# Second mixture: value products one block later, joins ahead of the copies, weight loads two at a time

## What is computed

```python
logits = x @ w_gate                      # x: 2304 tokens of 512
expert_idx = np.argmax(logits, axis=1)
gate_w = softmax(logits)[np.arange(N), expert_idx]
for e in range(E):                       # E = 8, hidden size F = 1024
    mask = expert_idx == e
    h = np.maximum(x[mask] @ w1[e], 0.0)
    out[mask] = gate_w[mask, None] * (h @ w2[e])
```

## Times and profile before

| | us |
|---|---|
| runs shown | 1200.71, 1200.39, 1196.43 |
| median | 1200.39 |
| profiled execution, its time | 1200.34 |
| its span in the trace | 1198.7 |
| PE busy | 1127.6 (94% of the span) |
| DVE busy | 591.6 (49%) |
| ACT busy | 289.2 (24%) |
| POOL busy | 311.6 (26%) |

### The profile page before, as it was taken

One profiled execution on the slowest core, in us unless ns is written; L12 is line 12 of the kernel. 1 busy time (PEld: TensorE's weight loads), 2 busy tenths in 40 slices (PEclk: granted clock), 3 DMA queues, 4 the chain that ended last, 5 costly groups with the idle time before them and its releaser, 6 DMA issues.

```text
span 1198.7 us, 19280 instructions
## 1 busy us (share of the span) xinstructions
PE 1127.6 (94%) x6726; PEld 984.0 (82%) x6726; DVE 591.6 (49%) x1158; ACT 289.2 (24%) x429; POOL 311.6 (26%) x191
## 2 busy tenths in 40 slices
PE   9999999999999999999999999999998889768874
PEld 6889988999999999999999998887776668656753
DVE  6345443222222222222232688885565877767764
ACT  3454334321111131111132111114501210221210
POOL 7200000510000060000033000016685640674640
PEclk9999999999999999999999999999998989888988
DMA  9233213300000120000031011117358734764844
GB/s 341 71 106 94 72 44 98 123 18 0 0 0 0 51 89 0 0 0 0 0 101 40 28 27 26 26 27 240 113 143 174 224 100 89 186 160 114 224 96 85
DMA packets 113315, 99.79 MB, mean 83 GB/s; under 512 B 72559, under 2 KB 97263, under 8 KB 113138
## 3 DMA queue, kind: packets, MB, share of 16 engines
q1 hardware_dynamic: 92498, 62.35, 20.8%
q10 hardware_dynamic: 16272, 25.21, 6.5%
q0 software_dynamic: 4496, 11.56, 3.2%
HBM read 73.48 MB, written 10.92 MB: 70 GB/s over the span
## 4 chain that ended last, share of the span: by engine, by line
PE 75%; DMA 9%; DVE 9%; issue 3%; SPq 2%; DVEq 1%; ACT 0%; POOL 0%; POOLq 0%
PE psum L1364 12%; PE psum L1366 12%; PE psum L1365 12%; PE psum L1410 11%; PE psum L1411 11%; PE psum L1412 11%; DMA h_planes_T<-h_planes 8%; DVE h_row_T L1181 2%; DVE h_planes L1173 2%; PE psum L1600 1%; DVE hThi L1191 1%; PE psum L1601 1%; PE psum L1602 1%; DVE psum L1183 1%; PE psum L1292 1%
## 5 line engine op out<-in xcount | busy, mean ns | idle before, releaser
L469 POOL TENSOR_TENSOR weights_r<-weights,weights_r 128x1024 fp32r<-128x1024 f32 x96 | 232.3, 2445 | 629.6 <-ACT weights_r L658 628.4
L1364 PE MATMUL psum<-xhi,weights_r 128*128 128x384 f32 (+1 forms) x772 | 260.0, 337 | 0.0
L1366 PE MATMUL psum<-xhi,weights_r 128*128 128x384 f32 (+1 forms) x772 | 257.8, 334 | 0.0
L1365 PE MATMUL psum<-xlo,weights_r 128*128 128x384 f32 (+1 forms) x772 | 257.7, 334 | 0.0
L1410 PE MATMUL psum<-weights_r,hhi 128*128 128x512 f32 x576 | 226.9, 394 | 0.0
L1412 PE MATMUL psum<-weights_r,hlo 128*128 128x512 f32 x576 | 224.8, 390 | 0.0
L1411 PE MATMUL psum<-weights_r,hhi 128*128 128x512 f32 x576 | 224.7, 390 | 0.0
L884 DVE SCALAR_TENSOR_TENSOR hlo<-psum,hhi 128x384 fp32r<-128x384 f32 x192 | 106.5, 557 | 219.3 <-ACT hhi L653 219.3
L653 ACT ACTIVATE hhi<-psum 128x384 fp32r<-128x384 f32 x192 | 94.5, 492 | 481.7 <-PE psum L1366 481.7
L658 ACT ACTIVATE weights_r<-weights 128x1024 fp32r<-128x1024 f32 x88 | 92.7, 1057 | 255.3 <-DMA weights<-in_moe_w 255.2
L1364 PEld LDWEIGHTS psum<-xhi,weights_r 128*128 128x128 f32 x772 | 144.9, 188 | 1.8
(11 more groups left out here) (187 smaller groups left out, 1176.0 us busy)
## 6 DMA issues: line engine op xcount, KB each, us to landing
weights<-in_moe_w SPq DMA_DIRECT2D x48, 512.0 KB, 3.9
weights<-in_moe_w ACTq DMA_DIRECT2D x48, 512.0 KB, 5.9
qkT<-in_qk SPq DMA_DIRECT2D x18, 512.0 KB, 4.1
v_rows<-in_v SPq DMA_DIRECT2D x18, 256.0 KB, 3.3
x_rows<-xfin SPq DMA_DIRECT2D x18, 256.0 KB, 4.3
wg_row<-in_gate_rows SPq DMA_DIRECT2D x1, 2048.0 KB, 7.3
h_planes_T<-h_planes SPq DMA_TRANSPOSE x46, 4.1
meta<-slot_table SPq DMA_DIRECT2D x26, 1.0 KB, 1.8
```

Source lines behind the costliest of these rows:

```text
L469: gp.tensor_tensor(rounded(set_, 1, c), raw(set_, c), rounded(set_, 0, c).bitcast(F32), ALU.subtract).then_inc(sem("w_lo"), 1)
L1364: mm(out_, ahi, bhi, start=(i == 0), stop=False)
L1365: mm(out_, ahi, blo, start=False, stop=False)
L1366: last = mm(out_, alo, bhi, start=False, stop=(i == n - 1))
```

## The change

PE: S(b-1) takes the place of S(b) after T(b+2), so that F(b+1) and T(b+2) stand one block further ahead of it. The first step of the loop is written out: S(1) is done in two halves around F(3). DVE: `join_h` works on the block whose copies were made in the round before, each join stands ahead of the copy of the same bank, each has its own half of `h_row_T`, and one ReLU of both halves (`relu_h`) follows after `take_xT`. The planes get other addresses. ACT issues two loads of four, and each of the other two after a `split_hi`. The branches for blocks that are not real follow the same shift.

```diff
-    h_planes_T = [tile(f"h_planes_T{i}", [P, 2, F // 2], U16, at["xfin"] + 2 * F * i) for i in range(2)]
-    h_row_T = tile("h_row_T", [P, F // 2], F32, at["xfin"] + 4 * F)
+    h_planes_T = [tile(f"h_planes_T{i}", [P, 2, F // 2], U16, at_)
+                  for i, at_ in enumerate((at["xfin"] + 4 * F, at["acc"] + 4 * NB * D + 4 * F))]
+    h_row_T = tile("h_row_T", [P, F], F32, at["xfin"])
...
-                        for c in range(i * NW // 2, (i + 1) * NW // 2):
+                        def load(c):
+
                             act.dma_start(raw(1 - u, c), source(v1, v2, source_e, c)).then_inc(raw_in[1 - u][c], 16)
-                        for c in range(i * NW // 2, (i + 1) * NW // 2):
+
+                        c0 = i * NW // 2
+                        load(c0)
+                        load(c0 + 1)
+                        for c in range(c0, c0 + NW // 2):
                             split_hi(1 - u, e0 // 2 + (1 if u == 0 else E1 + 1), c)
+                            if c + 2 < c0 + NW // 2:
+                                load(c + 2)
...
             def join_h(b, i):

-                n = seq(b) * 2 + i - 5
                 dve.wait_ge(h_planes_in[i], (seq(b) - 2) * 16)
-                words = h_row_T[:, :].bitcast(U16)
-                then(vec.reduce_max(words.rearrange("p (n h) -> p h n", h=2), h_planes_T[i][:, :, :].unsqueeze(3), axis=X),
-                     "h_joined", n)
-                then(vec.tensor_scalar(psum[:, HT_B + i, :], h_row_T[:, :], 0.0, None, ALU.max), "h_turned", n)
+                words = h_row_T[:, i * 512:(i + 1) * 512].bitcast(U16)
+                vec.reduce_max(words.rearrange("p (n h) -> p h n", h=2), h_planes_T[i][:, :, :].unsqueeze(3), axis=X)\
+                    .then_inc(sem("h_joined"), 1)
+
+            def relu_h(b):
+
+                dve.wait_ge(sem("h_joined"), seq(b) * 2 - 4)
+                vec.tensor_scalar(psum[:, HT_B:HT_B + 2, :], h_row_T[:, :].rearrange("p (i n) -> p i n", i=2), 0.0, None,
+                                  ALU.max).then_inc(sem("h_turned"), 1)
...
-            def block_step(b):
+            part_h(2, 0)
+            part_h(2, 1)
+            take_xT(3)
+
+            with dve.Fori(2, NR - 1) as b:
+                join_h(b, 0)
                 part_h(b + 1, 0)
+                join_h(b, 1)
                 part_h(b + 1, 1)
                 take_xT(b + 2)
-                join_h(b + 1, 0)
-                join_h(b + 1, 1)
-                take_result(b)
-                split_h(b + 1)
-
-            with dve.Fori(1, NR - 1) as b:
-                block_step(b)
+                relu_h(b)
+                take_result(b - 1)
+                split_h(b)
...
-            def block_step(b):
+            first_product(2)
+            transpose_rows(3)
+            second_product(1, range(0, FT // 2))
+            first_product(3)
+            transpose_rows(4)
+            second_product(1, range(FT // 2, FT))
+            for b in range(3, NR - 1):
                 first_product(b + 1)
                 transpose_rows(b + 2)
-                second_product(b)
-
-            for b in range(1, NR - 1):
-                block_step(b)
+                second_product(b - 1)
...
             def spare_step(b):

                 with pe.If(real > b + 1):
                     first_product(b + 1)
-                    second_product(b)
+                    second_product(b - 1)
                 with pe.Else():
                     pe.wait_ge(sem("hrow_ready"), seq(b) * 2 + 2)
                     pe.sem_inc(sem("l1a_psum"), 1)
                     pe.sem_inc(sem("l1b_psum"), 1)
-                    with pe.If(real > b):
-                        second_product(b)
-                    with pe.Else():
-                        skip_second(b)
+                    finish(b - 1)
...
+            finish(NB - 2)
+            finish(NB - 1)
```

More of the change, by code:

```diff
@@ L1176, in join_h @@
             def join_h(b, i):
-                n = seq(b) * 2 + i - 5
                 dve.wait_ge(h_planes_in[i], (seq(b) - 2) * 16)
-                words = h_row_T[:, :].bitcast(U16)
-                then(vec.reduce_max(words.rearrange("p (n h) -> p h n", h=2), h_planes_T[i][:, :, :].unsqueeze(3), axis=X),
-                     "h_joined", n)
-                then(vec.tensor_scalar(psum[:, HT_B + i, :], h_row_T[:, :], 0.0, None, ALU.max), "h_turned", n)
+                words = h_row_T[:, i * 512:(i + 1) * 512].bitcast(U16)
[5 more added lines that the diff above has]
+                                  ALU.max).then_inc(sem("h_turned"), 1)
             def split_h(b):
-                n = seq(b) * 2
                 src = psum[:, HT_B:HT_B + 2, :].rearrange("x b (r t) -> x (b r) t", t=P)
                 dve.wait_ge(sem("l2_psum"), seq(b) + 1)
[L1190 to L1193, removed]
+                dve.wait_ge(sem("h_turned"), seq(b) - 2)
+                vec.tensor_copy(hThi_r[:, :, :], src).then_inc(sem("hThi_ready"), 2)
+                dve.wait_ge(sem("hThi_ready"), seq(b) * 2 + 2)
                 vec.tensor_tensor(hTlo_r[:, :, :], src, hThi[:, :, :], ALU.subtract).then_inc(sem("hT_ready"), 2)
@@ L1232, in spare_step, with finish @@
                 with dve.If(real > b + 1):
+                    join_h(b, 0)
                     part_h(b + 1, 0)
+                    join_h(b, 1)
                     part_h(b + 1, 1)
                 with dve.Else():
-                    dve.wait_ge(sem("hT_ready"), seq(b) * 2 + 2)
-                    dve.sem_inc(sem("hrow_ready"), 2)
+                    with dve.If(real > b):
+                        join_h(b, 0)
+                        join_h(b, 1)
+                        dve.wait_ge(sem("h_joined"), seq(b) * 2 - 4)
+                        dve.sem_inc(sem("hrow_ready"), 2)
+                    with dve.Else():
+                        dve.sem_inc(sem("hrow_ready"), 2)
                 if ahead:
                     take_xT(b + 2)
[L1240 to L1244, removed]
+                finish(b)
+            def finish(b):
+                with dve.If(real > b):
+                    relu_h(b)
+                    take_result(b - 1)
+                    split_h(b)
                 with dve.Else():
-                    with dve.If(real > b):
-                        take_result(b)
+                    with dve.If(real > b - 1):
+                        take_result(b - 1)
                     with dve.Else():
-                        skip_result(b)
-                    dve.sem_inc(sem("hThi_ready"), 2)
-                    dve.sem_inc(sem("hT_ready"), 2)
+                        skip_result(b - 1)
             with dve.Fori(NR - 1, NB - 2) as b:
@@ L1255, in _ @@
             spare_step(NB - 2, False)
+            with dve.If(real > NB - 1):
+                join_h(NB - 1, 0)
+                join_h(NB - 1, 1)
+            finish(NB - 1)
             with dve.If(real > NB - 1):
@@ L1634, in skip_second, with finish @@
                 pe.sem_inc(sem("l2_psum"), 1)
+            def finish(b):
+                with pe.If(real > b):
+                    second_product(b)
+                with pe.Else():
+                    skip_second(b)
             def spare_step(b):
@@ L1644, in spare_step @@
                     pe.sem_inc(sem("l1b_psum"), 1)
-                    with pe.If(real > b):
-                        second_product(b)
-                    with pe.Else():
-                        skip_second(b)
-            for b in range(NR - 1, NB - 2):
-                transpose_rows(b + 2)
-                spare_step(b)
[L1653 to L1657, removed]
+                    finish(b - 1)
+            for b in range(NR - 1, NB - 1):
+                if b + 2 < NB:
+                    transpose_rows(b + 2)
+                spare_step(b)
+            finish(NB - 2)
+            finish(NB - 1)
 _INS = ["qk", "v", "moe_domain_probs", "moe_w1", "moe_w2", "moe2_w_gate", "gate_rows", "moe2_w1", "moe2_w2"]
```

## The result

The changed kernel takes 1165.72 us, the median of 4 runs (1159.01 to 1169.41), against 1200.55 (4 runs) of the kernel before: a ratio of 0.9715, with a 95% interval from 0.9651 to 0.9778. One of the four runs of the kernel before, 1214.70 us, was in a slower state of the chip and is left out of the ratio. The change makes the kernel faster by about 35 us, where 56 were forecast. The value lies 0.7 us above the wider range of the prediction (1130 to 1165) and 14 us above the narrower one (1136 to 1152). Run again later it took 1163.04 us (6 runs), ratio 0.967 (0.9628 to 0.9711).

What follows compares the result with a forecast made beforehand. PE's waits for split, join and transpose, and the slower clock behind them, bound the kernel. F(4) at 895.8, 16 blocks of 11.37, the 9.3 us stall and the end gave a 1142.5 us span, 1144 us forecast, range 1136 to 1152.

Steps and rivals of the forecast that it cites:

- DVE or the DMA as the part that sets the pace: Rival for the block rounds: DVE's round stays at 12.0 us, 1156 us, or late transposes give 1162; chance 0.22.
- no effect: Rival: split_h, still behind S(b-1), is late as before and S waits as before; 1200 us, chance 0.03.
- a slower kernel: Rival: weight supply becomes the bound and the end comes near 1290 us; chance 0.03 at or above 1200.
- No stall at F(20): Rival: ACT and POOL catch up before F(20), so 9.3 + 1.7 us go; 1133 us, chance 0.1.
- the stall: Forecast wait of F(20) for the weights of place 7, 9.3 us, range 7 to 12.
- The third rival, the weights: Loads in pairs make a group take 30 us, eleven groups 330 us; end near 1290, chance 0.03 at or above 1200.
- Four chunks then take ACT about 2 × (4.2 + 1.2) = 10.8 us: ACT's time for a group of four weight chunks loaded in pairs, 10.8 us instead of 10.4.
- 6 groups × 1.4 us = 8 us: Upper bound for slower weight groups in pairs, if all are on the path; nothing was taken outside F(20)'s stall.
- 2 in all for one or two that don't: Allowance of 2 us for one or two transposes beside weight loads not coming down to 5 to 8 us.
- Cover of 9.6 us: Time a transpose has to land before PE waits: 8.9 us, 9.6 with DVE's spare time.
- the 0 us that it was taken to give for late transposes: Value of the late-transpose term by the skill's shared-engines rule, 0 instead of the 2 us kept.
- the term of 1.7 us: Extra time of a product run at the lower clock behind a PE gap, 7.3 us against 5.58.

Runs made afterwards that it cites:

- four_loads: The changed kernel with all four loads of a group issued at once, as before the change; 1156.43 us, ratio 0.9633 to the kernel before.
- w1_first: The changed kernel with w1 chunks of the next place loaded, rounded and split ahead of w2 of the place before; 1162.91 us, ratio 0.970.
- paired_order_four: The changed kernel with refills in the order w1(e), w1(e+1), w2(e), w2(e+1), e even, and four loads at once; 1145.15 us, ratio 0.9525.
- the second trace: Trace of the changed kernel run once more with nothing altered; 1163.04 us.
- Late_gathers: The changed kernel with row gathers of blocks 13 to 24 issued behind the w1 chunks of place 2, not at the start; 1170.02 us, ratio 0.9729.

## Why the prediction was wrong

*The reading of what bounds the kernel was right*, and the pace too: PE without waits, DVE with time to spare, 11.37 us a block from S(3) to S(15). The wide ReLU took the 1.22 us of the row it was taken from. DVE's round has 10.3 us of work, for 10.7 said.

*The rivals.* DVE or the DMA as the part that sets the pace, no effect, and a slower kernel are all refuted by the same twelve blocks. "No stall at F(20)" is too; the stall was right, 10.1 us for 9.3, and 9.0 in four_loads. That it comes from the order of the lists was only argued then, and is shown by w1_first and paired_order_four, where it is gone. The third rival, the weights, was right in kind and far too large in size: it held at two places, not at all eleven groups.

*The first step that failed: "Four chunks then take ACT about 2 × (4.2 + 1.2) = 10.8 us".* It took the landing of a load with nothing beside it, 3.25 us, for all. But a pair is a chain of two landings, and each is exposed to what else is in flight. In the changed kernel the median landing was 4.9 us and the longest 11.9; the groups ahead of F(18) took 11.3, 12.9 and 18.6 us, and 11.8, 13.0 and 13.1 in the second trace. The two chunks that F(18) needs were said to be there 41.4 us after the end of S(11), with 4 to spare. They were there after 54.5, and after 47.8 in the second trace. With the slow clock this costs 9 to 11 us in the first trace and about 6 in the second. The bound that the text had for this, 6 groups × 1.4 us = 8 us, was given and then left out of the sum, and counted per group by the same short landing. Four_loads, where this wait is absent and the time about 7 to 9 us lower by the medians, shows it.

*The second step: "2 in all for one or two that don't".* This was the start. In the first trace it cost 8.5 us up to S(3): 2.1 at F(4) and 6.4 in the standstill, whose cause stays open. In the second trace S(3) is on time, and S(4) is 9.4 us late, behind late transposes and the slow clock. The text looked at transposes beside weight loads, and did not ask what the row gathers do to them. Before, the transposes around 899 landed after 9 and 10 us while the gathers ran; a gain of the change is that blocks run earlier, so now two blocks' transposes fall there, and w1 of place 2 is called up 2 to 10 us earlier, into the end of the same gathers. The longest landing was 13 us and more where 5 to 8 was said. Cover of 9.6 us, rightly worked out, wasn't enough. The runs with moved gathers support this: there the transposes landed after 3.0 to 7.9 us and F(6) waited for none, and with a right order besides S(4) begins at 924.3, which is the forecast's own sum (895.8 + 2.5 × 11.37). The proof is not complete, as one of the kernels with the gathers in place, paired_order_four, has no wait at F(6) either.

*What loads in pairs do.* They were expected to help the transposes at no cost. In the kernel before they do, by 13 us. In the changed one the block of cover already does that work, and by the medians pairs give some of it back. The change's two parts don't add up: −44 us for the later products with four loads, −13 for pairs alone, −35 together.

*The sentence of the page "DMA: Bandwidth & Descriptors" of the Trainium skill on a fixed cost for each transfer* (section "Anatomy of one DMA") pointed the right way: that a load waited for makes the supply longer, against the change. The page gives its 2.0 us for transfers that POOL issues, and these loads are issued by ACT. The prediction's estimate from it was 1.5 us; the groups became 0.4, 2.6 and 8.2 us longer than with four at once. The page's rule on shared DMA engines agrees with the traces: transposes took 13 and about 17 us, and loads 7 to 16, where they met. But the 0 us that it was taken to give for late transposes was refuted, as what was in flight beside them wasn't only what pairs could halve.

*The end.* The gaps before S(20) and S(21) are 3.5 and 3.4 us for 3.9. S(20) takes 8.2 us for 7.3, F(20) 8.0 for 7.1. The tail behind S(21) is 9.3 us for 7: its last transposes were issued at 1157.8 as expected, and the rest wasn't looked into.

*Still open* is what DVE and PE waited for between 898 and 910 us in the first trace: 3.6, 3.2 and some 1.5 us without a releaser that the profile names. It was in one of the six traces in which the gathers and the lists of DVE and PE stood as in the changed kernel, and cost no more than the late transposes did in the others. Late_gathers was made to test the gathers as its cause, but as the standstill is absent from the repeat of the unchanged program too, its absence there tells nothing.

## What to carry to other kernels

When a change takes one wait away everywhere, ask which supply ran in the shadow of that wait, and cost its chain at the landing times measured under load, not at the shortest one. Engines that serve refills from one list in order should have them in the order in which the buffers come free; here that was worth 11 us by the medians (1156.43 to 1145.15), behind which the way in which the loads are issued was no longer told apart. And a remedy for late transfers (fewer loads in flight) should be measured again once something else hides them: it won 13 us before, and cost about 7 to 9 after.

## What the runs showed of the hardware that was not expected

A DMA transpose of 256 KB, 3.1 us from issue to landing when alone, took 13 and about 17 us beside row gathers and one pair of 512 KB loads, and the loads beside it took 7 to 16 us: from 901 to 921 us the DMA engines moved 3.95 MB, 197 GB/s, where the first slice of the same execution has 349.

What the lower clock behind a gap of PE costs does not follow the length of the gap. In the ten traces the products behind nine gaps of 1.3 to 2.05 us took 5.6 us, as without a gap (those that a further wait broke up are not counted). Behind gaps of 2.2 to 3.8 us they took anything from 5.55 to 8.4 us: the same gap of 3.5 us before S(20) was followed by 5.6 to 8.4 us in eight traces. Behind gaps of 4.0 to 10.2 us they took 7.0 to 8.2 us. So the term of 1.7 us for one such product is a middle value, and each can be off by more than a microsecond.
